# First-layer start and four small-product tiles of an mLSTM plus two-layer feed-forward kernel: outputs by quarters of the columns, chunk 0's running sums as three bfloat16 parts

## The reference

```python
for t in range(S):
    m_new = maximum(f[t] + m, i[t]); f_stab = exp(f[t] + m - m_new); i_stab = exp(i[t] - m_new); m = m_new
    C = f_stab * C + i_stab * outer(v[t], k[t]);  n = f_stab * n + i_stab * k[t]
    y[t] = sigmoid(o[t]) * (C @ q[t]) / maximum(abs(n @ q[t]), 1)
x = y as [1536, 320]
x = (sigmoid(x @ w_gate) * (x @ w_val)) @ w_out            # layer one, d_ff = 1536
x = x / sqrt(mean(x * x) + 1e-6) * rms_g
out = (silu(x @ w_gate2) * (x @ w_val2)) @ w_out2          # layer two
```

## Time and profile before

| | |
|---|---|
| median of 3 runs | 448.79 us (448.45 to 449.05) |
| the profiled execution's own time | 448.17 us |
| its span in the trace | 446.3 us |
| PE busy | 441.9 us (99%) |
| DVE, ACT, POOL busy | 216.0, 183.9, 88.9 us |
| granted TensorE clock | 1.0 of full speed |

### The profile page before, as it was taken

One profiled execution on the slowest core, in us unless ns is written; L12 is line 12 of the kernel. 1 busy time (PEld: TensorE's weight loads), 2 busy tenths in 40 slices (PEclk: granted clock), 3 DMA queues, 4 the chain that ended last, 5 costly groups with the idle time before them and its releaser, 6 DMA issues.

```text
span 446.3 us, 10769 instructions
## 1 busy us (share of the span) xinstructions
PE 441.9 (99%) x4573; PEld 404.1 (91%) x4574; DVE 216.0 (48%) x481; ACT 183.9 (41%) x358; POOL 88.9 (20%) x138
## 2 busy tenths in 40 slices
PE   8999999999999999999999999999999999999997
PEld 5899999999999999988889988889988899888897
DVE  6876937854556456423432237561065630256510
ACT  7885377534663473124553144231033320233310
POOL 4567810112110200004556190000000000000000
PEclk9999999999999999999999999999999999999999
DMA  8984600331232114001333010000000000000000
GB/s 235 304 282 142 181 1 3 91 89 30 64 91 75 38 39 160 1 2 40 120 114 125 3 46 1 1 0 31 31 1 1 1 16 29 17 1 0 1 31 29
DMA packets 12032, 27.55 MB, mean 62 GB/s; under 512 B 1824, under 2 KB 6208, under 8 KB 11984
## 3 DMA queue, kind: packets, MB, share of 16 engines
q1 hardware_dynamic: 11728, 26.80, 19.7%
q10 hardware_dynamic: 256, 0.07, 0.1%
HBM read 24.81 MB, written 1.97 MB: 60 GB/s over the span
## 4 chain that ended last, share of the span: by engine, by line
PE 98%; DMA 1%; SPq 0%; ACT 0%; issue 0%
PE bank L1275 37%; PE bank L1226 21%; PE bank L1294 10%; PE bank L1296 9%; PE bank L1295 9%; PE bank L1164 3%; PE bank L1127 2%; PE bank L1047 2%; PE bank L1146 1%; PE bank L1083 1%; PE bank L1173 1%; DMA step<-in_qk_t 1%; PE bank L1114 0%; PE bank L1306 0%; PE bank L1321 0%; PE bank L1329 0%
## 5 line engine op out<-in xcount | busy, mean ns | idle before, releaser
L1275 PE MATMUL bank<-x_hi,wgv_hi 64*128 64x512 f32 x576 | 105.8, 388 | 0.0
L715 ACT ACTIVATE sg<-bank 128x256 f32<-128x256 f32 (+1 forms) x96 | 47.1, 492 | 128.6 <-PE bank L1275 82.6
L1275 PE MATMUL bank<-x_lo,wgv_hi 64*128 64x512 f32 x480 | 93.9, 386 | 0.0
L997 DVE TENSOR_TENSOR bank<-sg,bank 128x256 f32<-128x256 f32 (+1 forms) x96 | 53.8, 560 | 57.5 <-ACT sg L715 55.8
L1226 PE MATMUL bank<-x_hi,wgv_hi 128*128 128x256 f32 x288 | 80.6, 290 | 0.0
L1226 PE MATMUL bank<-x_lo,wgv_hi 128*128 128x256 f32 x288 | 77.8, 282 | 0.0
L1294 PE MATMUL bank<-wo_hi,h_hi 128*128 128x320 f32 x240 | 75.3, 314 | 0.0
L1275 PE MATMUL bank<-x_hi,wgv_lo 64*128 64x512 f32 x384 | 75.1, 386 | 0.0
L1296 PE MATMUL bank<-wo_hi,h_lo 128*128 128x320 f32 x240 | 74.1, 309 | 0.0
L1295 PE MATMUL bank<-wo_lo,h_hi 128*128 128x320 f32 x240 | 74.1, 309 | 0.0
L995 DVE TENSOR_TENSOR sg<-sg,bank 128x512 f32<-128x512 f32 x36 | 24.8, 688 | 83.0 <-ACT sg L715 83.0
(11 more groups left out here) (152 smaller groups left out, 554.8 us busy)
## 6 DMA issues: line engine op xcount, KB each, us to landing
step<-in_qk_t SPq DMA_DIRECT2D x24, 192.0 KB, 3.9
step<-in_vok SPq DMA_DIRECT2D x12, 324.0 KB, 4.2
step<-in_w_gv SPq DMA_DIRECT2D x6, 576.0 KB, 3.8
raw_x<-in_w_gv SPq DMA_DIRECT2D x4, 576.0 KB, 7.8
raw_p<-in_w_gv SPq DMA_DIRECT2D x4, 576.0 KB, 6.6
step<-in_vok SPq DMA_DIRECT2D x10, 160.0 KB, 5.7
raw_p<-in_w_o SPq DMA_DIRECT2D x3, 480.0 KB, 3.2
y<-y_tok SPq DMA_DIRECT2D x9, 160.0 KB, 1.8
```

The costliest lines, as they stand in the source:

```text
L715: act.activation(sg_view(n), g_view(n), ACT.Sigmoid).then_inc(sg_done, 1)
L997: dve.tensor_tensor(v_view(n), sg_view(n), v_view(n), ALU.mult).then_inc(hf_done, 1)
L1275: mm = pe.matmul(ps(n), w, x, start=own and (s, p) == (0, 0), stop=last and not own)
```

## The change

It has three parts. In tiles 2, 3, 10 and 11 the N step writes its 128 output rows by four matmuls of 32 stationary columns per head in place of two of 64, and K (in tiles 2 and 3) writes its 40 rows by two matmuls of 32 and 8 stationary columns in place of one of 40. At the start, `first_rows` replaces the first five row steps: m and f are computed for chunks 0 and 1 in one go (256 columns), the running sum of chunk 0 is stored as three bfloat16 parts, and PE adds it with bfloat16 matmuls over 80 rows whose stationary operand is a column of `sel_short`, for both batches before D of either. On POOL `ident` is built after the mask and its copies, and ACT fills the `sel` halves of both batches before it waits for `ident`.

```diff
--- before.py
+++ after.py
@@ -77,6 +77,8 @@
 VECTOR_AT = 5
 ONES_AT = 8
 
+BY_QUARTERS = [2, 3, NT - 2, NT - 1]
+
 SPLIT_AT = {0: [4], 2: [5], 3: [6], 4: [7], 5: [8], 7: [9], 8: [10], 9: [11]}
 
 
@@ -143,6 +145,7 @@
         num = sb("num", [P, HE], F32)
         ones = sb("ones", [R, P], F32)
         sel = sb("sel", [2 * Q, B, H], F32)
+        sel_short = sb("sel_short", [2 * Q + R, R], BF16)
         l_end = sb("l_end", [R, NJ, B, H], F32)
         ecol = sb("ecol", [P, NJ, R], F32)
         gcol = sb("gcol", [P, NJ, B, HG], F32)
@@ -156,7 +159,8 @@
         eps = sb("eps", [P, 1], F32)
 
 
-        l_row0 = first[1][:, 0:P]
+        l_row0 = first[1][:, 0:HALF].bitcast(BF16)
+        l_rest = inter[0:R, P:2 * P]
 
         hide = num[:, 0:2 * P].rearrange("p (u t) -> p u t", t=P)
         wexp = [t[:, 0:H * P].rearrange("p (h t) -> p h t", t=P) for t in tails]
@@ -468,10 +472,7 @@
                 link(pool.affine_select(out=sel[:, :, :], in_=sel[:, :, :], compare_op=ALU.not_equal, fill=1.0,
                                         base=-Q * n, pattern=[[-H, B], [-1, H]], channel_multiplier=1))
             pool.memset(half_neg[:, :], -0.5).then_inc(consts, 1)
-            link(pool.memset(ident[:, :], 0.0))
-            pool.affine_select(out=ident[:, :], in_=ident[:, :], compare_op=ALU.not_equal, fill=1.0, base=0,
-                               pattern=[[-1, P]], channel_multiplier=1).then_inc(consts, 1)
-            pool.wait_ge(consts, 2)
+            pool.wait_ge(consts, 1)
 
             link(pool.memset(hide, 0.0))
             link(pool.affine_select(out=hide, in_=hide, compare_op=ALU.is_ge, fill=NEG, base=-HALF,
@@ -493,6 +494,10 @@
                 pool.wait_ge(hide_done, done)
 
             hide_of(1, 2)
+            link(pool.memset(ident[:, :], 0.0))
+            pool.affine_select(out=ident[:, :], in_=ident[:, :], compare_op=ALU.not_equal, fill=1.0, base=0,
+                               pattern=[[-1, P]], channel_multiplier=1).then_inc(consts, 1)
+            pool.wait_ge(consts, 2)
 
 
             lows, splits = [0, 0], [0, 0]
@@ -685,8 +690,9 @@
             for b in range(B):
                 hs = slice(H * b, H * b + H)
                 act.activation(d_rhs[0:HALF, hs, :], sel[0:HALF, b, :].unsqueeze(2).to_broadcast([HALF, H, P]), ACT.Copy)
-                if b == 0:
-                    act.wait_ge(consts, 2)
+            act.wait_ge(consts, 2)
+            for b in range(B):
+                hs = slice(H * b, H * b + H)
                 act.activation(d_rhs[HALF:P, hs, :].rearrange("p r (u t) -> p r u t", u=2),
                                ident[HALF:P, HALF:P].unsqueeze(1).unsqueeze(1).to_broadcast([HALF, H, 2, HALF]),
                                ACT.Copy).then_inc(fill_done, 1)
@@ -793,53 +799,51 @@
             def lhs(p0, j0, j1, w):
                 return d_lhs[p0:p0 + R, j0:j1, :, w * HALF:w * HALF + HALF]
 
+            def first_rows():
+
+                hi = 2 * P
+                dve.wait_ge(gates_in, 16)
+                link(dve.tensor_tensor_scan(m_r[:, 0:hi], f_r[:, 0:hi], i_r[:, 0:hi], NEG, ALU.add, ALU.max))
+                dve.memset(f_r[:, 0:1], 0.0)
+                link(dve.tensor_tensor(f_r[:, 1:hi], f_r[:, 1:hi], m_r[:, 0:hi - 1], ALU.add))
+                link(dve.tensor_tensor(f_r[:, 1:hi], f_r[:, 1:hi], m_r[:, 1:hi], ALU.subtract))
+
+                link(dve.tensor_tensor_scan(l_r[:, 0:P], ones[:, :], f_r[:, 0:P], 0.0, ALU.mult, ALU.add))
+                dve.tensor_copy(l_row0[0:R, :], l_r[:, 0:P]).then_inc(high_done, 1)
+                dve.wait_ge(high_done, 1)
+                link(dve.tensor_tensor(l_rest, l_r[:, 0:P], l_row0[0:R, :], ALU.subtract))
+                link(dve.tensor_copy(l_row0[Q:Q + R, :], l_rest))
+                dve.tensor_tensor(l_row0[2 * Q:2 * Q + R, :], l_rest, l_row0[Q:Q + R, :],
+                                  ALU.subtract).then_inc(rows_done, 1)
+
+                link(dve.tensor_tensor(i_r[:, 0:hi], i_r[:, 0:hi], m_r[:, 0:hi], ALU.subtract))
+                link(dve.tensor_tensor(i_r[:, 0:P], i_r[:, 0:P], l_r[:, 0:P], ALU.subtract))
+                link(dve.tensor_copy(d_lhs[0:R, 0:1, :, :], twice(i_r[:, 0:P])))
+                dve.tensor_tensor(d_lhs[Q:Q + R, 0:1, :, :], twice(i_r[:, 0:P]),
+                                  d_lhs[0:R, 0:1, :, :].bitcast(F32), ALU.subtract).then_inc(lhs0_done, 1)
+
+                dve.tensor_tensor_scan(l_r[:, P:hi], ones[:, :], f_r[:, P:hi], 0.0, ALU.mult, ALU.add).then_inc(sums_done, 1)
+                dve.wait_ge(sums_done, 1)
+                link(dve.tensor_tensor(i_r[:, P:hi], i_r[:, P:hi], l_r[:, P:hi], ALU.subtract))
+
             def rows(part, sub):
                 j0, j1 = PARTS[part]
                 lo, hi = j0 * P, j1 * P
                 cs = slice(lo, hi)
                 ls = slice(j0 % LR * P, j0 % LR * P + hi - lo)
                 if sub == 0:
-
-                    if part == 0:
-                        dve.wait_ge(gates_in, 16)
-                        link(dve.tensor_tensor_scan(m_r[:, cs], f_r[:, cs], i_r[:, cs], NEG, ALU.add, ALU.max))
-                        dve.memset(f_r[:, 0:1], 0.0)
-                        link(dve.tensor_tensor(f_r[:, 1:hi], f_r[:, 1:hi], m_r[:, 0:hi - 1], ALU.add))
-                        link(dve.tensor_tensor(f_r[:, 1:hi], f_r[:, 1:hi], m_r[:, 1:hi], ALU.subtract))
-                    else:
-                        link(dve.tensor_tensor_scan(m_r[:, cs], f_r[:, cs], i_r[:, cs], m_r[:, lo - 1:lo],
-                                                    ALU.add, ALU.max))
-                        link(dve.tensor_tensor(f_r[:, cs], f_r[:, cs], m_r[:, lo - 1:hi - 1], ALU.add))
+                    link(dve.tensor_tensor_scan(m_r[:, cs], f_r[:, cs], i_r[:, cs], m_r[:, lo - 1:lo], ALU.add, ALU.max))
+                    link(dve.tensor_tensor(f_r[:, cs], f_r[:, cs], m_r[:, lo - 1:hi - 1], ALU.add))
                 elif sub == 1:
-                    if part:
-                        link(dve.tensor_tensor(f_r[:, cs], f_r[:, cs], m_r[:, cs], ALU.subtract))
+                    link(dve.tensor_tensor(f_r[:, cs], f_r[:, cs], m_r[:, cs], ALU.subtract))
 
                     for j in range(j0, j1):
                         js = slice(j * P, (j + 1) * P)
-                        last = dve.tensor_tensor_scan(l_r[:, js], ones[:, :], f_r[:, js], 0.0, ALU.mult, ALU.add)
-                    if part == 0:
-                        link(last)
-                        dve.tensor_copy(l_row0[0:R, :], l_r[:, cs]).then_inc(high_done, 1)
-                        dve.tensor_tensor(i_r[:, cs], i_r[:, cs], m_r[:, cs], ALU.subtract)
-                        dve.wait_ge(high_done, 1)
-                        dve.tensor_tensor(l_row0[Q:Q + R, :], l_r[:, cs], l_row0[0:R, :].bitcast(F32),
-                                          ALU.subtract).then_inc(rows_done, 1)
-                        dve.wait_ge(rows_done, 1)
-                        link(dve.tensor_tensor(i_r[:, cs], i_r[:, cs], l_r[:, cs], ALU.subtract))
-                    elif part == 1:
-                        last.then_inc(sums_done, 1)
-                        link(dve.tensor_tensor(i_r[:, cs], i_r[:, cs], m_r[:, cs], ALU.subtract))
-                        dve.wait_ge(sums_done, 1)
-                        link(dve.tensor_tensor(i_r[:, cs], i_r[:, cs], l_r[:, cs], ALU.subtract))
+                        dve.tensor_tensor_scan(l_r[:, js], ones[:, :], f_r[:, js], 0.0, ALU.mult, ALU.add)
                 elif sub == 2:
                     if part > 1:
                         link(dve.tensor_tensor(i_r[:, cs], i_r[:, cs], m_r[:, cs], ALU.subtract))
                         link(dve.tensor_tensor(i_r[:, cs], i_r[:, cs], l_r[:, cs], ALU.subtract))
-                    if part == 0:
-                        link(dve.tensor_copy(d_lhs[0:R, j0:j1, :, :], twice(i_r[:, cs])))
-                        dve.tensor_tensor(d_lhs[Q:Q + R, j0:j1, :, :], twice(i_r[:, cs]),
-                                          d_lhs[0:R, j0:j1, :, :].bitcast(F32), ALU.subtract).then_inc(lhs0_done, 1)
-                        return
                     for w in range(2):
                         high = dve.tensor_copy(lhs(0, j0, j1, w), keys(i_r[:, cs], w))
                     if part > 1:
@@ -963,13 +967,13 @@
 
             dve.memset(inter[:, 0:1], 0.0).then_inc(idle_in, 1)
             dve.memset(ones[:, :], 1.0)
-            dve.memset(l_row0.bitcast(F32), 0.0)
+            dve.memset(l_row0, 0.0)
             dve.memset(d_lhs[0:HALF, 0, :, :].bitcast(F32), 0.0)
             link(dve.memset(d_lhs[0:HALF, 1, :, :].bitcast(F32), 1.0))
-            for sub in range(3):
-                rows(0, sub)
-            for sub in range(2):
-                rows(1, sub)
+            dve.wait_ge(consts, 1)
+            for p0, p1 in ((0, 2 * Q), (2 * Q, 2 * Q + R)):
+                dve.tensor_copy(sel_short[p0:p1, :], sel[0:p1 - p0, :, :].rearrange("p b h -> p (b h)"))
+            first_rows()
             for n in range(B):
```

(22 more changed lines are left out.)

## The result

The kernel after takes 451.28 us in the median of seven runs (451.03 to 454.47), the one before 448.45 (448.36 to 449.05) beside it. The ratio is 1.0077 with an interval of 1.0053 to 1.0102: slower, on the other side of the forecast and outside its range. The profiled execution took 451.25 us, its span is 449.4, against 446.3 before. Four of the seven runs took 451.03 to 451.28 us at a mean granted clock of 0.999 or 1.0; the other three, 452.55 to 454.47, had 0.992 to 0.996.

The account below looks back on a forecast made before the run. PE, carrying 98% of the chain, was taken to bound the kernel. From the profiled 448.17 us, 0 for start and tiles 2 and 3 and -0.66 for tiles 10 and 11 gave 447.5, 448.1 as a median; range 447.0 to 449.4.

Parts of the forecast that it names:

- N by quarters: N step on PE: 16 rounds of 37.5 ns, 0.60 us instead of 0.93, so 0.33 less per tile.
- K by quarters: K step of tiles 2 and 3: still 8 rounds, now of four records, 37.5 ns each, so zero change.
- 0.30 more in each tile: Upper bound on the cost of K by quarters in tiles 2 and 3, in us; the lower bound was 0.05 less.
- Rounds of four: N on PE: with 32 columns a round is four records run together, taken as 37.5 ns, bounds 30.8 to 75.
- tiles 10 and 11: Late N steps, where the chain is PE to the end: 2 x 0.33 = 0.66 us is kept.
- B: Rival for matmuls by quarters: each record has a floor of 15.3 ns whatever its columns; 449.4 us, chance 0.13.
- C: Rival for matmuls by quarters: only two column parts of 32 run at once, 75 ns a round; 450.5 us, chance 0.12.
- Tiles 2 and 3 pay nothing: Early N steps: their 0.66 us is waited away at 51.94 us for POOL's chunk 11; 0, give or take 0.25.
- as fixed at 51.82: End of POOL's output-weight chunk 11, in us, taken as unmoved by the change, with 0.25 us allowed either way for contention.
- The start: New first row steps: layer one 0.07 us later, bounds 0.1 earlier to 0.5 later, covered by room from tiles 2 and 3.
- The sum: Whole kernel: 448.17 + 0 (start, tiles 2 and 3) - 0.66 = 447.5 us, 448.1 as a median.

Follow-up runs that it names:

- experiment 4: The kernel after with K of tiles 2 and 3 whole again, N still by quarters: 448.44 us, ratio 0.9998 to the kernel before.
- experiment 2: The kernel before with N of tiles 10 and 11 alone by quarters, old start: 448.0 us, ratio 0.9988.
- experiment 3: The kernel before with N and K of tiles 2 and 3 alone by quarters, old start: 453.69 us, ratio 1.0111.
- experiment 6: The kernel before with N of tiles 2, 3, 10 and 11 by quarters, K whole, old start: 448.14 us, ratio 0.999.
- eleven: The kernel before with N of tiles 2, 3, 10, 11 by quarters, K whole, POOL's hold removed, SP holding later loads back: 447.36 us, ratio 0.9974.
- experiment 1: The kernel after with no tile by quarters, only the new start left: 448.91 us, ratio 1.0009 to the kernel before.
- twelve: The same as eleven, but with N by quarters in tiles 10 and 11 only: 447.82 us, ratio 0.9979.
- experiment 8: Experiment 4 with POOL no longer waiting for DVE's split of chunk 7 before its own of chunk 6: 449.94 us, ratio 1.0043.
- experiment 10: The kernel after with SP holding loads of tile 4 and later until N of tile 3 is done: 452.57 us, ratio 1.0075.
- experiment 7: The kernel before with N of tiles 2 to 11 by quarters, K whole, old start: 449.79 us, ratio 1.0022.
- experiment 5: The kernel after with four early idle matmuls replaced by 32 one-column matmuls: 449.31 us, ratio 1.0017 to the kernel before.
- experiment 9: The kernel after with seven early idle matmuls replaced by 64 one-column matmuls: 450.37 us, ratio 1.0043 to the kernel before.

## Why the prediction was wrong

**The step that failed** is in "N by quarters" and "K by quarters": both priced a step by its rounds in the array and took it as given that PE has its instructions. Under "K by quarters" the text says "8 rounds, now of four records [...] 37.5 ns as before, zero". K's rounds are as priced (0.43 us for 0.44), and those 32 more records a tile fill the block: with them the two stops cost 1.6 us (30.49 to 32.20, less the usual 0.12) and 2.1 us (45.36 to 47.48), without them nothing (experiment 4). The bound of "0.30 more in each tile" was a bound on the array. None of the rivals was this one. The numbers for it were in reach: the page of before has the instruction queue with as many transfers as PE has blocks of 256 records, and I, K and N together were 160 instructions in 2 us already. But no trace of before has a stop, so its size could not have come from there.

**Rounds of four: right.** With four column parts the array runs four records at a time, with all 128 rows in use. N's 64 records run in 16 rounds of about 37 ns, 0.60 us, and what is left of the 0.75 lies between its last start and the first layer-one matmul (0.13 us; 0.16 in the kernel before). So tiles 10 and 11 give 0.60 against 0.66 forecast (experiment 2: 0.5 in the median). In tiles 2 and 3 the gain depends on K. I measure from K's last matmul to the first of layer one behind N: 1.06 us in the kernel before. With K by quarters (experiment 3, tile 2) it is 0.77, so 0.29 less, near the 0.33 forecast; N starts 0.03 behind K, as before. With K whole (experiments 4, 6 and 11) it is 0.88, so 0.18 less: N then starts 0.13 behind K, the change of shape that the prediction saw K by quarters avoid. Rivals B and C fall; C needed 1.3 us or more for an N.

The Trainium skill, "TensorE: Matmul & The Clock Gate", section "Wait — 56ns, not 53.3ns?", has about 25 ns between starts as the least. The traces disagree, where four parts of the array are in use: 64 records in 0.75 us are 12 ns each.

**Tiles 2 and 3 pay nothing: right,** and by the mechanism named. In experiments 1, 2, 4 and 6, which have no stop, PE waits 0.5 to 0.7 us at about 52 us for POOL's chunk 11, and in eleven and twelve, where that chunk is earlier, it doesn't. The number was too exact, though. POOL's end was taken "as fixed at 51.82"; it came at 52.50 and 52.53 in experiments 2 and 6, since chunk 6 landed at 31.0 in place of 30.29 and the whole chain DMA, ACT, DVE, POOL moved with it. The 0.03 us of wait in the trace of before was one draw. That 51.82 and 51.94 lay so close was luck; the mechanism was not.

**The start: mis-sized.** The forecast was 0.07 later for layer one, within -0.1 to +0.5; it is 0.30 later, and experiment 1 has 0.4 us in the median. DVE came out as priced: `rows_done` at 6.79 (forecast 6.90), `lhs0_done` at 8.31 (8.3):

```profile
6.51 0.28 DVE L816 TENSOR_TENSOR first<-inter,first 16x128 bf16<-16x128 f32 x1
...
7.90 0.41 DVE L822 TENSOR_TENSOR d_lhs<-fi_r,d_lhs 16x256 fp32r<-16x256 f32 x1
```

PE's sixteen bfloat16 matmuls took 1.00 us in the chain, 0.063 each and not 0.08, and were done before `lhs0_done`; it changed nothing. `ident` was ready at 5.26 us, not 4.5, and ACT waited 1.27 us for it, not 0.4; its copies were done at 7.29, still ahead of D, so that changed nothing either. What slipped is the exponentials on ACT:

```profile
8.93 1.09 ACT L644 ACTIVATE tail<-bank 128x512 f32<-128x512 f32 x2 [1.64 <-PE bank L1339]
...
12.86 0.83 ACT L673 ACTIVATE step<-step 128x320 f32<-128x320 f32 x2
```

The exponentials start 0.73 later (8.20 before) and not 0.43. PE's D started at 8.42, 0.12 after the forecast, and the rest is a misreading of the chain of before: I took its 7.87 for the start of D of tile 0, where the chain had only come to it; PE's timeline of before has that D at 7.71,

```profile
7.71 0.69 PE L1329 MATMUL bank<-d_rhs,d_lhs 128*128 128x256 f32 x4
```

so that D is 0.71 later. From there the order held: the sigmoids 0.73 later (12.86, before 12.13), POOL's row after them at 13.41, ending at 14.81 for 14.51.

```profile
13.41 1.40 POOL L579 TENSOR_TENSOR step<-step,rden 128x320 f32<-128x320 f32 x2 [0.81 <-ACT step L673]
```

How the 0.4 us of experiment 1 reach the end is not shown. In its trace PE waits 0.50 us, to 53.05, for POOL's chunk 11, so this chunk was last there and not the start of layer one; chunk 6 had landed at 31.45, beside 31.00 in experiment 2. With the new start it landed between 30.69 and 31.79 in six traces, with the old one between 30.29 and 31.72 in seven: from these it can't be read that the start moves it.

**The sum.** Forecast 0 + 0 - 0.66. Measured in the traces: start +0.15 at the S of tile 2, N of tiles 2 and 3 about -0.4, stops +3.7, tiles 10 and 11 -0.60; that is 2.85, of 3.1. With the stops gone (experiment 4) the change is worth 0.1 us in the medians (448.44 beside 448.53), not to be told from nothing: the late tiles' 0.5 less the start's 0.4. The 0.62 us that the forecast put between the profiled execution and the median came from three runs; by the seven beside the result it is 0.28.

## What to carry to other kernels

Count an engine's instructions per microsecond, not only their lengths. When a step is cut into more and smaller matmuls, look where some 250 PE records fall within 2 to 3 us (256 in I, K and N stopped PE here; 224, with K whole, did in experiment 8 and did not in 4, 6 and 11), and suspect missing instructions behind an "issue" stop between two matmuls of one group. The remedy is fewer records in the dense stretch; here it was K whole, which costs 0.1 us a tile on PE. Before a gain is counted, follow the nearest chain that PE has no part in, and take its end from more than one trace.

## What the hardware showed that was not expected

- PE's instructions come in transfers of 16 KB, one for about every 250 PE records: 36 transfers for 9,147 records, 37 for 9,467, 38 for 9,523, 39 for 9,787. Stops came at 935 records (to within two) and again 504 later in experiments 3 and 10 and in the kernel after, whatever the lines there. The brackets of the windows view leave out the records of PE's own sequencer, such as its waits. Counted with them, the ten stops of more than 1 us in these traces lie at 448, 960, 1,472 and 4,288 records, to within one, and three shorter ones in experiment 7 (0.11 to 0.27 us, ending at 79.66, 123.44 and 155.65) at 2,240, 3,776 and 4,800: each is 192 more than a multiple of 256. From the start of the transfer's packet to PE going on it was 2.2 to 2.9 us in the ten stops. That the stops are missing instructions is inferred from these counts and from experiments 4, 5 and 9, which moved or removed them; no row names it.
- What decides when such a transfer begins was not settled, but the traces speak for the data in the queues. PE passed the border at 1,216 (same count) at 42.6 to 43.6 us in the kernel before and in experiments 4, 8, 10, 11 and 12, and the next packet began at 48.26, 44.76, 48.30, 45.83, 44.08 and 44.56. In 11 and 12 the DMA engines were nearly idle from 43 to 45 us (shares of 0.00 to 0.09), in 10 busy until 45.8, in 8 busy from 43 to 48 (0.68 to 1.13 in each microsecond). Against it, in the kernel before a microsecond at 0.42 (44 to 45) let no packet through. Density alone is enough too: ahead of the stop of 1.18 us in experiment 7 the DMA share was 0.06, the packet began 0.7 us behind the border, and PE was through the next 256 records 2.1 us behind that border.
- After stops of 2.47 us and more (experiments 3, 8 and 10) the granted clock fell to 0.50 for 3.4 us, and after the one of 1.83 us in experiment 9, which other short waits surround, for 6.8 us. After the stop of 1.93 us in the profiled execution of the kernel after it stayed at 1.0, but three of that kernel's seven runs, which have no trace, had a lower mean clock (0.992 to 0.996) and took 1.3 to 3.2 us more than the median. In experiment 3 the lower clock added 1.48 us, about as much as a stop.
- Small DMA differences move the landing of chunk 6 between 30.29 and 31.79 us from kernel to kernel. In the kernel before and in experiments 1, 2, 4, 6 and 7 POOL's last chunk starts 18.4 to 18.5 us behind it, in the kernel after and in experiments 3 and 5, which have a stop, 19.5 to 19.7.
